# Moving four attention products of the third row of blocks from the serial opening into the first dense steps

## The chip, the cores and the metric

The program runs on one core of one Trainium2 chip. The metric is device time in microseconds (us), from one launch to its end, lower is better. The core has a matrix engine (TensorE, PE in the profile, with its weight loads as PEld), a vector engine (DVE), a scalar engine (ACT), GpSimd (POOL), SyncE (SP), which here issues most of the transfers, and 16 DMA engines. Each engine runs its own instructions in the order in which they are written and waits on semaphores for the others. SBUF is the on-chip memory, PSUM the memory that PE writes to.

## The reference, cut to what matters

Three layers follow one another: windowed attention with a bias by distance, a feed-forward layer with SiLU, and a layer of eight experts in which each token goes to one. The change lies in the first layer and in the opening of the second.

```python
def _attn_ref(q, k, v, n_global, n_local):           # q, k, v: (4, 8, 768, 64)
    scores = scale * np.matmul(q, k.transpose(0, 1, 3, 2))
    ...
    scores = np.where(keep, scores + bias, -1000000000.0)
    scores = scores - np.max(scores, axis=-1, keepdims=True)
    a = np.exp(scores)
    a = a / (np.sum(a, axis=-1, keepdims=True) + 1e-09)
    return np.matmul(a, v)                            # the "values" of this text

def _moe_ref(x, w_in, w_out):                         # x: (3072, 512)
    h = x @ w_in                                      # "up"
    g = h * (1.0 / (1.0 + np.exp(-h)))
    return (g @ w_out)                                # "down"
```

## The kernel before, in words

**Rows and units.** The 3,072 tokens are 24 rows of 128 (six per batch entry). A row has four units, each a pair of heads; unit `u` belongs to row `u // 4`. A unit goes through five stages: `score` (PE: q times k into `qk_ps`), `shift`, `exp` and `scale_probs` (DVE, ACT, DVE: the softmax), `turn` (PE transposes the probabilities into `pt_ps`), `keep_turned` (ACT copies them to a slot of `probs_t`), and `value` (PE multiplies them with the row's v in `v_w` into the one bank `o_ps`, called `notes_ps` in the rows). When a row's four values are there, `replace_x` (DVE, waits for `values_done`), `round_x` (ACT) and `rest_x` (DVE) make `x_high` and `x_low`, a high and a low part of the row. `o_ps` is single, so the first value of a row waits until `rest_x` of the row before has read it.

**Dense chunks.** Two rows are a group, and a group has 16 chunks `m`; for each PE does `up(m)` (12 matmuls of 256 columns), and two chunks later `down(m)` (6 of 512). Between them ACT does `half_tanh(m)` and `round_g(m)`, DVE `twice_silu(m)`, and POOL `rest_g(m)`, which makes `g_low`; `down(m)` waits for `g_low`. In the first group the weights are also split: a chunk's weights arrive in one of four buffers `w_raw`, ACT makes `w_high`, and DVE (even chunks) or POOL (odd ones) makes the low parts, which release the buffer for the next load.

**Order.** All engines walk over steps `n`. Steps 0 to 11 (`LEAD` is 12) are the serial opening, one unit a step with little to cover its waits. From step 12 on each step has two chunks, `m = 2(n - 12)` and the next, and `up` runs two chunks ahead. Scores come two units at a time in even steps; the four values of a row come together in every fourth step, at n = 16, 20 and so on (`valued_in`). Nothing but this written order decides what an engine does next. Steps 14 and 16, which the prediction speaks of, begin with the scores of units 14 and 15 and of units 16 and 17; step 16 has the values 12 to 15, those of row 3.

**v and the queue of SP.** `v_w` holds one row's v, so row 3's v can be loaded only when the values of row 2 (units 8 to 11) are done: the load goes in two halves, `load_v(row)` waits for `values_done` before each. SP issues all loads of q, k, v and weights one after another in the order of its own steps, and a load that waits holds up those behind it. Row 1's v lies in slots 2 and 3 of `probs_t` (`second_v`), so units before 12 use only slots 0 and 1.

Of the kernel before, what the change touches and what calls it, by code (L numbers as in the profile page):

```python
# [168 lines left out]
def attention_and_silu(nc, block, sems_ctx, first, tables, last_down, notes_ps, qk_rows, v_win, limits, beyond, weights, gate_rows,  # L169
# [6 lines left out]
    PAIRS = H // 2  # L176
# [8 lines left out]
    LEAD = 12  # L185
# [8 lines left out]
    with ExitStack() as ctx:  # L194
        def sb(name, shape, dt=F32):
            return ctx.enter_context(nc.sbuf_tensor(name, shape, dt))
# [4 lines left out]
        def sem(name):  # L201
            return sems_ctx.enter_context(nc.semaphore(name))
# [9 lines left out]
        probs_t = sb("probs_t", [P, PAIRS, 4, P])  # L212
# [34 lines left out]
        values_done = sem("values_done")  # L247
# [21 lines left out]
        def reached(eng, semaphore, value):  # L269
            if value > 0:  # L270
                eng.wait_ge(semaphore, value)

        def unit_there(u):
            return 0 <= u < UNITS
# [7 lines left out]
        def row_of(u):  # L282
            return u // PAIRS, u % PAIRS

        def keys_of(row):
            return (half, window) if row % tiles else (P // 2, P)
# [8 lines left out]
        def scored_in(n):  # L295
            return [u for u in (n, n + 1) if unit_there(u)] if n >= LEAD and n % 2 == 0 else []

        def valued_in(n):
            return [u for u in range(n - PAIRS, n) if unit_there(u) and u >= LEAD - 2] if n >= LEAD and n % PAIRS == 0 else []

        def turned_behind(m):
            n, k = LEAD + m // 2, m % 2
# [9 lines left out]
        def x_row_in(n):  # L312


            if n < LEAD:
                return row_ended(n, 3)
            return row_ended(n, 1) if n % 2 == 0 else None

        def scores_of(u):
            at = 256 if u >= LEAD and u % 2 else 0  # L320
            return qk_ps[:, :, at:at + keys_of(u // PAIRS)[1]]

        def turned_of(u):
            return probs_t[:, u % (2 if u < LEAD else PAIRS), :, :]

        def v_of(row):
            return second_v if row == 1 else v_w
# [4 lines left out]
        def row_ended(n, lag):  # L332

            u = n - lag
            return u // PAIRS if unit_there(u) and u % PAIRS == PAIRS - 1 else None
# [10 lines left out]
        def split_in(n):  # L346


            if LEAD - 4 <= n < LEAD - 2:
                return (n - LEAD + 4,)  # L350
            f = 2 * (n - LEAD + 2)
            return (f, f + 1) if LEAD - 1 <= n and f < FC else ()
# [10 lines left out]
        def rows_of(grp):  # L363

            start = sum(PER_GROUP[:grp])
            return start // E, start
# [27 lines left out]
        @block.sync  # L394
        def _(sp):
            def load_qk(row):

                reached(sp, qk_done, (row - 1) * PAIRS)
                used = P + keys_of(row)[1]
                sp.dma_start(qk_t[:, row % 2, :, 0:used], qk_rows[row, :, :, 0:used]).then_inc(qk_in[row % 2], 16)  # L400

            def load_v(row, halves=(0, 1)):


                part, _ = keys_of(row)
                for k in halves:
                    reached(sp, values_done, (row - (2 if row == 2 else 1) if row > 1 else -1) * PAIRS + (k + 1) * PAIRS // 2)
                    pairs = slice(k * PAIRS // 2, (k + 1) * PAIRS // 2)
                    sp.dma_start(v_of(row)[0:part, pairs, :, :, :], v_win[row, 0:part, pairs, :, :, :])\
                        .then_inc(v_in[row % 2 * 2 + k], 16)  # L410

            def load_weights(f):

                reached(sp, w_low_ready[f % 2], (f - RAW) // 2 + 1)
                sp.dma_start(w_raw[:, f % RAW, :], weights[f, :, :]).then_inc(w_in_sbuf[f % RAW], 16)


            sp.wait_ge(scores_ready, 2)
            load_qk(1)
            load_v(1)  # L420
            load_qk(2)
            load_v(2, (0,))
            load_weights(0)
            sp.wait_ge(bias_ready, H // 2 - 1)
            sp.wait_ge(pair_bias_ready, 1)
            load_weights(1)
            load_v(2, (1,))
            for f in range(2, RAW):
                load_weights(f)
            for n in range(UNITS + 4):  # L430
                row = row_ended(n, 0)
                if row is not None and 0 < row < ROWS - 2:
                    load_qk(row + 2)
                for f in split_in(n):
                    if f + RAW < FC:
                        load_weights(f + RAW)
                if row is not None and 1 < row < ROWS - 1:
                    load_v(row + 1)
                grp = (n - LEAD) // (FC // 2)
                if n > LEAD and (n - LEAD) % (FC // 2) == FC // 4 and 0 < grp < G - 1:  # L440

                    sp.wait_ge(dots_done, grp * GT * E)
                    sp.wait_ge(x2_stored, grp * 16)
                    chunk, _ = rows_of(grp)
                    sp.dma_start(x2[:, :, :], weights[chunk:chunk + 2, :, C * P:].rearrange("f p c -> p f c"))\
                        .then_inc(w_out_in, 16)
                if n == LEAD + FC // 2 - 2:
                    for k in range(2):
                        sp.wait_ge(w_low_ready[k], FC // 2)
                    sp.dma_start(gate_all, gate_rows.partition_broadcast(P)).then_inc(gate_all_in, 16)  # L450
# [54 lines left out]
        def _(pe):  # L505
# [29 lines left out]
            def value(u):  # L535
                row, pair = row_of(u)
                part, _ = keys_of(row)
                if pair % (PAIRS // 2) == 0:
                    pe.wait_ge(v_in[row % 2 * 2 + pair // (PAIRS // 2)], 16 * (row // 2 + 1))
                if pair == 0:  # L540
                    reached(pe, x_low_ready, row)
                pe.wait_ge(probs_t_ready, u + 1)
                for c in range(2):
                    for a in range(2):
                        last = nc.tensor.matmul(o_ps[a * D:(a + 1) * D, pair, :], v_of(row)[0:part, pair, a, c, :],
                                                turned_of(u)[0:part, a * 2 + c, :], start=c == 0, stop=c == 1)
                last.then_inc(values_done, 1)
# [46 lines left out]
            def unread_products(count):  # L594

                for _ in range(count):
                    nc.tensor.matmul(up_ps[:, 1, 256:256 + P], ident[:, :], ident[:, :], start=True, stop=True)

            for n in range(STEPS):
                if n < LEAD:  # L600


                    score(n)
                    unread_products({0: 8, 1: 3}.get(n, 0))
                    turn_last = (n - 3) % PAIRS != 0
                    if n == 2:
                        unread_products(5)
                    if n >= 2 and not turn_last:
                        turn(n - 2)
                    if n == PAIRS + 3:  # L610
                        unread_products(4)
                    if n >= 3:
                        value(n - 3)
                    if n >= 2 and turn_last:
                        turn(n - 2)
                    unread_products({2: 3, 3: 2}.get(n, 0))
                for u in scored_in(n):
                    score(u)
                for u in valued_in(n):
                    value(u)  # L620
                for m in chunks_of(n):
                    if chunk_there(m + AHEAD):
                        up(m + AHEAD)
                    if chunk_there(m) and m < LAST:
                        down(m)
                    elif chunk_there(m):
                        if m == LAST + 1:
                            pe.wait_ge(x2_ready, (G - 1) * GT)
                        last_down.products(pe, nc, downs_ahead(m))
                        last_logits(m)  # L630

                    if m == -2:
                        turn(LEAD - 2)
                        value(LEAD - 3)
                    if m == -1:
                        turn(LEAD - 1)
                    if turned_behind(m) is not None:
                        turn(turned_behind(m))
# [7 lines left out]
        def _(act):  # L646
# [9 lines left out]
            def keep_turned(u):  # L656

                row, _ = row_of(u)
                part, _ = keys_of(row)
                reached(act, values_done, u - 1 if u < LEAD + 2 else u - PAIRS + 1)  # L660
                act.wait_ge(transposed, u + 1)
                nc.scalar.activation(turned_of(u)[0:part, :, :], pt_ps[0:part, :, :], ACT.Copy)\
                    .then_inc(probs_t_ready, 1)
# [40 lines left out]
            for n in range(STEPS):  # L704
# [7 lines left out]
                row = x_row_in(n)  # L712
# [1398 lines left out]
```

## Time and profile before

| what | value |
|---|---|
| median of 3 runs | 1054.82 us (1053.95 to 1056.28) |
| the profiled execution's own time | 1054.26 us |
| its span | 1052.6 us |
| PE busy | 1029.0 us, 98% |
| DVE, ACT, POOL busy | 69%, 43%, 40% |
| clock granted to PE over the span | 0.998 of full speed |

The span is the time from the first to the last instruction on the core; the profiled execution took 1.66 us more than it. PE's share is high because its matmuls are pipelined and count as busy from issue to end. The other engines have idle time in plenty, and it costs only where PE waits for them.

### The profile page before, as it was taken

Reading aid. Unit: us, or ns where it says so; the run is one execution under the profiler, and the core shown is the slowest. Engines: PE = TensorE matmul, PEld = TensorE weight load, DVE = VectorE, ACT = ScalarE, POOL = GpSimd, SP = SyncE. Lnnn points to the kernel's source line nnn. Section 1 sums busy time; section 2 is a strip of 40 time slices with the busy share of each in tenths; the row PEclk is TensorE's granted clock in tenths of the full one; section 3 lists DMA queues with packets and bytes.
Section 4 is the critical chain, followed back from the end, with each engine's and each line's share of the span. In section 5 each row is a group of like instructions: output and inputs, shape, how many; then the busy total and the mean of one; then the engine's idle time right before and its main releaser. Section 6 shows DMA issues by size and latency. Waiting matters only on the chain. (4 is left out here: it accounts for less than half of the span.)

```text
span 1052.6 us, 20243 instructions
## 1 busy us (share of the span) xinstructions
PE 1029.0 (98%) x7331; PEld 888.2 (84%) x7331; DVE 721.7 (69%) x2535; ACT 457.1 (43%) x1170; POOL 425.2 (40%) x474
## 2 busy tenths in 40 slices
PE   8899999999999999999999999998999999999998
PEld 7688888888888888888888888986778878878997
DVE  6764767777777777877777786765767868766210
ACT  5775444444544454444444443320434334334442
POOL 1363222222222222222222134312776777678773
PEclk9999999999999999999999999999999999999999
DMA  6653212222221222122222111003154254335320
GB/s 185 225 205 125 75 60 77 77 70 66 78 67 54 76 77 67 59 70 65 71 77 78 39 50 31 21 1 140 72 213 156 96 198 178 126 138 191 140 110 31
DMA packets 25827, 103.41 MB, mean 98 GB/s; under 512 B 3024, under 2 KB 5072, under 8 KB 23536
## 3 DMA queue, kind: packets, MB, share of 16 engines
q0 software_dynamic: 9824, 58.99, 15.6%
q1 hardware_dynamic: 15904, 43.13, 12.4%
q8 instruction: 59, 0.97, 0.4%
q14 instruction: 40, 0.33, 0.1%
HBM read 89.52 MB, written 12.85 MB: 97 GB/s over the span
## 5 line engine op out<-in xcount | busy, mean ns | idle before, releaser
L476 POOL TENSOR_TENSOR g_low<-g,g_high 128x256 fp32r<-128x256 f32 x176 | 142.6, 811 | 433.0 <-ACT g_high L690 433.0
L576 PE MATMUL up_ps<-x_high,w_high 128*128 128x256 f32 x768 | 227.7, 297 | 0.0
L576 PE MATMUL up_ps<-x_low,w_high 128*128 128x256 f32 x768 | 215.3, 280 | 0.0
L576 PE MATMUL up_ps<-x_high,w_in_low 128*128 128x256 f32 x768 | 215.2, 280 | 0.0
L690 ACT ACTIVATE g_high<-g 128x256 fp32r<-128x256 f32 x176 | 73.5, 418 | 211.1 <-DVE g L872 126.6
L576 PEld LDWEIGHTS up_ps<-x_high,w_high 128*128 128x128 f32 x768 | 144.6, 188 | 12.0 <-issue 9.1
L872 DVE SCALAR_TENSOR_TENSOR g<-g,up_ps 128x256 f32<-128x256 f32 x192 | 79.9, 416 | 98.2 <-ACT g L682 97.8
L576 PEld LDWEIGHTS up_ps<-x_low,w_high 128*128 128x128 f32 x768 | 144.7, 188 | 2.2
L576 PEld LDWEIGHTS up_ps<-x_high,w_in_low 128*128 128x128 f32 x768 | 144.4, 188 | 0.0
L830 DVE CUSTOM_DVE_ANT_0 product<-x,w_raw 128x512 bf16<-128x512 f32 x176 | 141.2, 802 | 3.0
L590 PE MATMUL down_ps<-w_high,g_high 128*128 128x512 f32 x352 | 138.8, 394 | 0.9 <-POOL g_low L476 0.9
L590 PE MATMUL down_ps<-w_high,g_low 128*128 128x512 f32 x352 | 139.4, 396 | 0.0
L590 PE MATMUL down_ps<-w_out_low,g_high 128*128 128x512 f32 x352 | 138.8, 394 | 0.0
L842 DVE CUSTOM_DVE_ANT_0 product<-x,w_raw 128x512 bf16<-128x512 f32 x128 | 103.9, 811 | 33.9 <-DMA x<-weights 31.9
L652 ACT ACTIVATE probs<-probs,neg_max 128x232 f32<-128x232 f32 (+1 forms) x184 | 85.1, 464 | 47.0 <-DVE neg_max L770 46.9
L682 ACT ACTIVATE g<-up_ps 128x256 f32<-128x256 f32 x192 | 72.9, 380 | 74.7 <-PE up_ps L576 55.3
L1537 POOL TENSOR_TENSOR w_low<-w_raw,w_high 128x512 fp32r<-128x512 f32 x64 | 82.0, 1292 | 46.1 <-ACT w_high L1740 43.9
L1676 PE MATMUL eup_ps<-ex_high,w_high 128*128 128x384 f32 x256 | 91.6, 358 | 1.1 <-DVE ex_low L1991 1.1
L1676 PE MATMUL eup_ps<-ex_high,w_low 128*128 128x384 f32 x256 | 86.1, 336 | 0.0
L1676 PE MATMUL eup_ps<-ex_low,w_high 128*128 128x384 f32 x256 | 86.1, 336 | 0.0
L1522 POOL TENSOR_TENSOR w_low<-w_raw,w_high 128x512 fp32r<-128x512 f32 x64 | 80.1, 1289 | 2.6 <-ACT w_high L1733 2.5
L590 PEld LDWEIGHTS down_ps<-w_high,g_low 128*128 128x128 f32 x352 | 66.1, 188 | 15.3
(244 smaller groups left out, 1984.0 us busy)
## 6 DMA issues: line engine op xcount, KB each, us to landing
qk_t<-qk_rows SPq DMA_DIRECT2D x20, 720.0 KB, 4.2
v_w<-v_win SPq DMA_DIRECT2D x38, 232.0 KB
w_raw<-weights SPq DMA_DIRECT2D x16, 512.0 KB, 4.6
x_rest<-x_any POOLq DMA_DIRECT2D x24, 256.0 KB, 2.9
x_rows<-x POOLq DMA_DIRECT2D x12, 512.0 KB, 3.2
x<-weights SPq DMA_DIRECT2D x10, 512.0 KB, 3.6
w_raw<-gate_rows SPq DMA_DIRECT2D x1, 2048.0 KB, 8.0
qk_t<-qk_rows SPq DMA_DIRECT2D x3, 512.0 KB, 3.9
```

The source lines that it names most:

```text
L476: pool.tensor_tensor(g_low_of(u), g[:, u % 2, :], g_high_of(u).bitcast(F32), ALU.subtract)\
L576: last = nc.tensor.matmul(up_ps[:, u % 2, 0:GT * P], a[:, f, w], x[:, grp % 2, c, :], start=k == 0, stop=k == 3 * C - 1)
L590: last = nc.tensor.matmul(down_ps[:, t, :], a[:, m % 2, t * P:(t + 1) * P], x[:, f, :], start=f == 0 and k == 0, stop=f == FC - 1 and k == 2)
L652: nc.scalar.activation(probs_of(u)[:, a, 0:width], probs_of(u)[:, a, 0:width], ACT.Exp, bias=neg_max[:, u % 3, a:a + 1], scale=-1.0, accum ...
L682: nc.scalar.activation(g[:, u % 2, :], up_ps[:, u % 2, 0:GT * P], ACT.Tanh, scale=0.5)\
L690: nc.scalar.activation(g_high_of(u), g[:, u % 2, :], ACT.Copy).then_inc(g_high_ready, 1)
L830: v.tensor_tensor_reduce(out=product[:, :], in0=x2[:, t, :], in1=gate_all[:, e, :], scale=1.0, scalar=0.0, op0=ALU.mult, op1=ALU.add, accu ...
L842: v.tensor_tensor_reduce(out=product[:, :], in0=x2[:, k // E - chunk, :], in1=gate_all[:, k % E, :], scale=0.5, scalar=0.0, op0=ALU.mult, ...
L872: v.scalar_tensor_tensor(g[:, u % 2, :], g[:, u % 2, :], 1.0, up_ps[:, u % 2, 0:GT * P], ALU.add, ALU.mult).then_inc(g_ready, 1)
L1522: pool.tensor_tensor(w1_low[:, f, :], w1_raw[:, p % 2, f, :], w1_high[:, f, :].bitcast(F32), ALU.subtract).then_inc(w1_low_ready, 1)
L1537: pool.tensor_tensor(w2_low[:, f, :], w2_raw[:, f, :], w2_high[:, f, :].bitcast(F32), ALU.subtract).then_inc(w2_low_ready, 1)
L1676: last = nc.tensor.matmul(up_ps[:, f % UP_BANKS, 0:CAP], w[:, f, c * P:(c + 1) * P], x[:, c, :], start=k == 0, stop=k == 3 * C - 1)
```

## The change

In the opening, the values of row 2 (units 8 to 11) were computed at steps 11, 11, 12 and 12, each soon after its probabilities were turned. They are now computed two at a time in the dense steps: units 8 and 9 at step 12, units 10 and 11 at step 14. What makes `x_high` and `x_low` of row 2 follows in step 14 instead of step 12. Units 8 to 11 use all four slots of `probs_t`, so that each has its own. SP's load of v for row 3 moves from step 11 to step 14, behind the weights that are issued there, since the values it waits for now come later.

```diff
         def valued_in(n):
-            return [u for u in range(n - PAIRS, n) if unit_there(u) and u >= LEAD - 2] if n >= LEAD and n % PAIRS == 0 else []
+            if n in (LEAD, LEAD + 2):
+
+                return [n - PAIRS, n - PAIRS + 1]
+            return [u for u in range(n - PAIRS, n) if unit_there(u)] if n > LEAD and n % PAIRS == 0 else []
...
-            if n < LEAD:
+            if n < LEAD or n == LEAD + 2:
                 return row_ended(n, 3)
-            return row_ended(n, 1) if n % 2 == 0 else None
+            return row_ended(n, 1) if n > LEAD and n % 2 == 0 else None
...
-            return probs_t[:, u % (2 if u < LEAD else PAIRS), :, :]
+            return probs_t[:, u % (2 if u < LEAD - PAIRS else PAIRS), :, :]
...
                 for f in split_in(n):
                     if f + RAW < FC:
                         load_weights(f + RAW)
+
+                row = row_ended(n, 3) if n == LEAD + 2 else row if n > LEAD else None
                 if row is not None and 1 < row < ROWS - 1:
                     load_v(row + 1)
...
-                    if n >= 3:
+                    if 3 <= n < LEAD - 1:
                         value(n - 3)
...
                     if m == -2:
                         turn(LEAD - 2)
-                        value(LEAD - 3)
...
-                reached(act, values_done, u - 1 if u < LEAD + 2 else u - PAIRS + 1)
+                reached(act, values_done, u - 1 if u < LEAD - 2 else max(u - PAIRS + 1, 2 * PAIRS))
                 act.wait_ge(transposed, u + 1)
```

Line numbers behind the first edit grow by 3 to 5. In the rows below, `value` is L545 before and L550 after, `up` L576 and L581, `load_v` L409 and L412, `load_weights` L415 and L418, `load_qk` L400 and L403.

PE, from the turning of unit 9 to the `up` of chunk 2, before, with what the first instruction of each piece waits for (`up` of chunks 0 and 1 stand behind the first two values; rows left out are the other matmuls of each piece and the turns of units 10 and 11):

```order
L531 MATMUL pt_ps<-ident,probs 116x128 [waits probs_t_ready,scaled]
...
L545 MATMUL notes_ps<-probs_t,v_w 64x128 [waits probs_t_ready,x_low_ready,v_in0]
...
L576 MATMUL up_ps<-x_high,w_high 128x256 [waits w_low_ready0,x_low_ready]
...
L545 MATMUL notes_ps<-probs_t,v_w 64x128 [waits probs_t_ready]
...
L576 MATMUL up_ps<-x_high,w_high 128x256 [waits w_low_ready1]
...
L518 MATMUL qk_ps<-qk_t 128x232 [waits scores_ready,qk_in1]
...
L545 MATMUL notes_ps<-probs_t,v_w 64x128 [waits probs_t_ready,v_in1]
...
L576 MATMUL up_ps<-x_high,w_high 128x256 [waits g_ready,w_low_ready0]
```

The scores of units 12 to 15 and the values behind them on PE in the changed kernel, in the same manner (the first four rows open step 12, the last four step 14):

```order
L523 MATMUL qk_ps<-qk_t 128x232 [waits scores_ready,qk_in1]
...
L550 MATMUL notes_ps<-probs_t,v_w 64x128 [waits probs_t_ready,x_low_ready,v_in0]
...
L550 MATMUL notes_ps<-probs_t,v_w 64x128 [waits probs_t_ready]
...
L581 MATMUL up_ps<-x_high,w_high 128x256 [waits g_ready,w_low_ready0]
...
L523 MATMUL qk_ps<-qk_t 128x232 [waits scores_ready]
...
L550 MATMUL notes_ps<-probs_t,v_w 64x128 [waits probs_t_ready,v_in1]
...
L550 MATMUL notes_ps<-probs_t,v_w 64x128 [waits probs_t_ready]
...
L581 MATMUL up_ps<-x_high,w_high 128x256 [waits g_ready,w_low_ready0]
```

No value stands between a turn and an `up` any more; two values follow the scores in step 12, and two more in step 14, where none stood.

SP, from the load of row 3's q and k on, before (the x6 are the weights of chunks 8 to 13):

```order
L400 DMA qk_t<-qk_rows 128x1440
L415 DMA w_raw<-weights 128x1024 x2
L400 DMA qk_t<-qk_rows 128x1440
L415 DMA w_raw<-weights 128x1024 x2
L409 DMA v_w<-v_win 116x512 x2
L415 DMA w_raw<-weights 128x1024 x6
L400 DMA qk_t<-qk_rows 128x1440
L415 DMA w_raw<-weights 128x1024 x2
```

SP in the changed kernel, the same place:

```order
L403 DMA qk_t<-qk_rows 128x1440
L418 DMA w_raw<-weights 128x1024 x2
L403 DMA qk_t<-qk_rows 128x1440
L418 DMA w_raw<-weights 128x1024 x8
L412 DMA v_w<-v_win 116x512 x2
L403 DMA qk_t<-qk_rows 128x1440
L418 DMA w_raw<-weights 128x1024 x2
```

The two halves of row 3's v (116 partitions of 512 elements each) stood ahead of the weights of chunks 8 to 13 and now stand behind them, between the weights of chunk 13 and the q and k of row 5.

DVE in step 14 of the changed kernel, from `replace_x` of row 2 to the low parts of the weights of chunk 8:

```order
L806 COPY_PREDICATED notes_ps<-beyond,x_rest 128x512
L785 TENSOR_SCALAR inv<-sums 128x2
L787 RECIPROCAL inv<-inv 128x2
L790 TENSOR_SCALAR probs<-probs,inv 128x232 x2
L785 TENSOR_SCALAR inv<-sums 128x2
L787 RECIPROCAL inv<-inv 128x2
L790 TENSOR_SCALAR probs<-probs,inv 128x232 x2
L813 TENSOR_TENSOR x_low<-notes_ps,x_high 128x4x128
L876 SCALAR_TENSOR_TENSOR g<-g,up_ps 128x256
L798 TENSOR_TENSOR w_in_low<-w_raw,w_high 128x512
```

The first row and the `x_low` row stood in step 12 before; in step 14 they are new, both ahead of `g` of chunk 6.

## Rows read from the trace of the kernel before

**Rows 1.** The page: busy time of the engines, share of the span, instructions

```profile
PE 1029.0 (98%) x7331; PEld 888.2 (84%) x7331; DVE 721.7 (69%) x2535; ACT 457.1 (43%) x1170; POOL 425.2 (40%) x474
```

**Rows 2.** Busy time by stretch: length, busy PE, PEld, DVE, ACT, POOL, clock, DMA share, GB/s

```profile
35.00:44.00 9.00, 7.43 (x72) 5.97 (x70) 6.62 (x26) 6.27 (x16) 2.00 (x2) 1.00 0.71 254
44.00:60.00 16.00, 16.00 (x108) 13.89 (x105) 10.62 (x30) 11.48 (x28) 11.23 (x11) 1.00 0.60 182
60.00:80.00 20.00, 20.00 (x155) 17.64 (x154) 12.29 (x36) 14.46 (x32) 11.71 (x12) 1.00 0.52 191
...
110.00:640.00 530.00, 529.33 (x3889) 461.46 (x3888) 401.69 (x1322) 242.66 (x697) 136.65 (x178) 1.00 0.20 66
```

**Rows 3.** Timeline of PE, steps 11 and 12: start, length, instruction, idle before it

```profile
34.86 0.66 PE L545 MATMUL notes_ps<-probs_t,v_w 116*64 116x128 f32 x8 [0.78 <-issue]
...
37.56 0.65 PE L531 MATMUL pt_ps<-ident,probs 128*116 128x128 f32 x4 [0.43 <-DVE probs L786]
...
43.56 0.66 PE L545 MATMUL notes_ps<-probs_t,v_w 116*64 116x128 f32 x8 [1.14 <-ACT probs_t L662]
...
44.14 0.39 PE L576 MATMUL up_ps<-x_high,w_high 128*128 128x256 f32 x1
...
45.70 0.50 PE L590 MATMUL down_ps<-w_high,g_high 128*128 128x512 f32 x1
```

**Rows 4.** Timeline of POOL from 44.3 us: `rest_g` of chunk 0

```profile
44.47 1.18 POOL L476 TENSOR_TENSOR g_low<-g,g_high 128x256 fp32r<-128x256 f32 x1
```

**Rows 5.** Timeline of PE at the start of step 14, then of step 16

```profile
56.59 1.05 PE L518 MATMUL qk_ps<-qk_t 64*128 64x232 f32 x8
57.58 0.39 PE L576 MATMUL up_ps<-x_high,w_high 128*128 128x256 f32 x1
...
69.89 1.05 PE L518 MATMUL qk_ps<-qk_t 64*128 64x232 f32 x8
70.87 1.97 PE L545 MATMUL notes_ps<-probs_t,v_w 116*64 116x128 f32 x32
72.77 0.38 PE L576 MATMUL up_ps<-x_high,w_high 128*128 128x256 f32 x1
```

**Rows 6.** Timeline of DVE and POOL, steps 14 and 16

```profile
61.34 0.42 DVE L872 SCALAR_TENSOR_TENSOR g<-g,up_ps 128x256 f32<-128x256 f32 x1
...
64.77 1.29 POOL L463 TENSOR_TENSOR w_out_low<-w_raw,w_high 128x512 fp32r<-128x512 f32 x1
...
72.95 0.70 DVE L802 COPY_PREDICATED notes_ps<-beyond,x_rest 128x512 f32<-128x512 int32 x1 [0.50 <-PE notes_ps L545]
...
76.17 0.41 DVE L872 SCALAR_TENSOR_TENSOR g<-g,up_ps 128x256 f32<-128x256 f32 x1
```

**Rows 7.** Timeline of SP: issues of weights, q and k, and v

```profile
49.99 16.42 SPq L415 DMA_DIRECT2D w_raw<-weights  x6
66.45 0.43 SPq L400 DMA_DIRECT2D qk_t<-qk_rows  x1
...
72.00 1.15 SPq L409 DMA_DIRECT2D v_w<-v_win  x2
```

**Rows 8.** The weights' transfers of 512 KB between 38 and 80 us

```profile
DMA to landing us min/median/max: 3.4/4.0/5.1
```

**Rows 9.** DMA from 72 to 82 us in 40 slices, then 74.8 to 80.5 us

```profile
DMA  9988999961122222222222252222200000000000
...
DMA  2114122122232222222227222222222200000000
...
q1 hardware_dynamic: 210, 0.41, 20.3%
```

**Rows 10.** PE around its only drop of clock: timeline, then columns as Rows 2

```profile
727.66 0.75 PE L1619 MATMUL route_ps<-ids,one_hot 128*32 128x24 bf16 x24 [2.76 <-issue]
...
725.00:730.00 5.00, 2.34 (x32) 2.34 (x33) 1.46 (x8) 0.00 (x0) 2.34 (x4) 0.94 0.76 246
730.00:735.00 5.00, 5.00 (x24) 5.00 (x23) 2.81 (x11) 0.00 (x0) 3.74 (x4) 0.72 0.95 392
```

## The prediction

> **What bounds the kernel now.** The page comes first: PE is busy for 1029.0 us, 98% of the span, the next engine, DVE, for 69% [rows 1]. The busy time by stretch then shows where PE has slack: from 44 to 80 us PE is busy all the time, and from 110 to 640 us it lacks 0.67 us of 530 [rows 2]. So whatever moves PE's work in the opening shifts all that follows by the same amount, up or down, and nothing behind it can take a delay back. The question is when PE gets through step 16, where the order of its work is again the same in both kernels.
>
> The timeline of PE in steps 11 and 12 has three waits: 0.78 us before the value of unit 8 (it waits for `x_low` of row 1, since `o_ps` is single), 0.43 us before the turn of unit 10, and 1.14 us before the value of unit 11, whose turned probabilities ACT has not yet copied. Then `up` of chunk 2 starts at 44.14 us and `down` of chunk 0 at 45.70 us [rows 3].
>
> **What the change removes.** Four values leave the stretch before 44.14 us, 0.66 us of PE for each [rows 3], and with them the wait of 1.14 us. But each saving ends at the next wait. `up` of chunk 0 waits for the same `x_low` as the value did, so it starts about 0.6 us earlier; the turn of unit 10 then waits for DVE, which is untouched, and starts at 37.56 us as before. From there the value of unit 9 (0.6 us) and the 1.14 us fall away, and units 8 and 9 stand where 10 and 11 stood, with no wait. `up` of chunk 2 therefore starts some 1.7 us earlier, near 42.4 us. Behind it stands `down` of chunk 0, which waits for `g_low` from POOL: that instruction runs from 44.47 to 44.47 + 1.18 = 45.65 us, and `down` starts at 45.70 us [rows 3, 4]. What POOL does before hangs on ACT and DVE, which wait for none of the removed values. So nearly all of the 1.7 us turns into a wait for POOL. Bounds: at least 0 (POOL as now); at most 0.45 us, if the 1.18 us shrink to 0.73 us, where DVE's work beside it changes. I take 0.1 us gained, near the lower end, since DVE will scale probabilities beside it instead of replacing x.
>
> **What it adds.** Two values in step 14. From the scores to the first `up` it takes 57.58 - 56.59 = 0.99 us there now, and 72.77 - 69.89 = 2.88 us in step 16, where four values stand between [rows 5]. Two values are half of the difference, 0.95 us, on a PE with no idle time. The other two only fill the place of units 10 and 11.
>
> **What it moves, and what is late next.** The load of row 3's v is the step that I take to decide. Before, it was issued in step 12. Now SP issues it in step 14 behind the weights of chunk 13. That load waits until POOL has made the low parts of chunk 9's weights, at 64.77 + 1.29 = 66.06 us [rows 6], and the row after it on SP (q and k of row 5) shows the queue free at 66.45 us [rows 7]. So v would be issued at 66.45 us, plus what DVE and POOL are later. They are later, because `replace_x`, 0.70 us, and `x_low` now stand ahead of `g` of chunk 6. In step 14 now, `g` starts 61.34 - 56.59 = 4.75 us after the scores; in step 16, with four values and both instructions, 76.17 - 69.89 = 6.28 us [rows 5, 6]. The difference of 1.53 us holds four values; two values less give between 0.6 and 1.5 us, and I take 1.0. Issue of v: 66.45 + 1.0 = 67.45 us, the second half some 0.4 us behind.
>
> How long does it take? By size alone it would be quick: 512 KB of weights land in 3.4 to 5.1 us [rows 8], and each half of v has 232 KB. The next load of v says otherwise. It was issued from 72.00 us [rows 7]. In the DMA view from 72 us the engines are nearly all busy until about 74.2 us with what was queued before, and then one fifth of them until about 79.5 us; from 74.8 us on the queue has 210 packets, no more than 20.3% of 16 engines, that is three to four of them, and the last slice with traffic ends near 79.8 us [rows 9]. So both halves together have landed some 7.8 us after the issue, and the first, taken as half of the 5.6 us from 74.2 us, about 5 us after it. The Trainium skill (DMA: Bandwidth & Descriptors, Why a DMA increments its semaphore by 16 and not by 1) says that a transfer is split over the largest number of engines, at most 16, that divides its slowest dimension. For 116 partitions that makes 4 engines; the trace agrees with its 20.3%.
>
> When does PE want it? The values of units 12 to 15 start at 70.87 us [rows 5]; shifted by -0.1 + 0.95 that is 71.72 us. The first half lands at 67.45 + 5 = 72.45 us or later: a wait of 0.7 us, up to 1.6 us if it takes 5.9. Unit 14 needs the second half, which PE reached at 70.87 + 0.98 = 71.85 us before. It lands at 67.45 + 7.8 = 75.25 us at the earliest, so PE is 3.4 us later there than before. Something comes on top: the semaphore, and row 5's q and k and the x of POOL's queue, which are in flight at the same time, while almost nothing ran beside the load that I read. Bounds for the second half: 7.8 us (as read) and 9.3 us (1.5 us on top, a fifth more). I take 8.6 us. PE is then at 67.45 + 8.6 - 71.85 = 4.2 us later than before, and as the order is the same from there, it stays so.
>
> **The sum.** -0.1 (opening) + 0.95 (two values) + 3.35 (waits for the halves of v) = +4.2 us. Against the profiled execution's own 1054.26 us that is 1058.5 us; the median of the runs shown is 0.56 us above that execution, so 1059.0 us for the median. The cost of all other edits is nothing: the four slots add no instruction, and ACT's new wait for 8 values is fulfilled before each copy. If SP's load of v came in time, that cover would make the sum +0.85 us.
>
> **Rivals.**
> - *v lands in time.* Then no wait stands in step 16: +0.4 to +1.3 us, 1055.2 to 1056.1, which 0.2% (2.1 us, about what a measurement tells from no change) doesn't tell from the kernel before. For it speak the 3.4 to 5.1 us of the larger weights [rows 8]. It is decided by the second half: it must land within 71.72 + 0.98 - 67.45 = 5.2 us of the issue. Against it stand the 7.8 us of the next load. This is the rival on the other side. If the wait of 1.14 us also paid off in full because POOL came earlier, it would be -1.6 + 0.95 = -0.65 us, still within 0.2%; faster than that needs something that no row shows.
> - *v is late, but by little.* SP gets to the load earlier (the 1.0 us does not come about, since DVE has idle time in step 14), and the halves run beside each other. PE would be later by 75.25 - 1.0 - 71.85 = 2.4 us: 1057.2.
> - *The wait costs clock as well.* PE's granted clock fell below full speed in the stretch from 725 us on, in which PE had been idle for 2.76 us before 727.66 us: 0.94 in the first five microseconds, 0.72 in the next [rows 10]. That is 0.3 + 1.4 = 1.7 us lost. In step 16 two waits of 1 to 2.5 us stand with only one short piece of work between; if the clock fell there as well, the sum would be 4.2 + 1.7 = +5.9 us, 1060.7. Against it: from 35 to 44 us PE was idle for 1.57 of 9 us and kept the full clock [rows 2], and in the changed kernel it is busy from 46 us to the first of these waits.
>
> **How the numbers follow.** Late v as summed, with its bounds +3.3 to +5: 0.63. Late by little, +1 to +3.3: 0.17, half of it over 2.1 us. Clock as well, +5 to +7: 0.06. v in time: 0.12. Faster by another way: 0.02. So slower by over 0.2% has 0.63 + 0.08 + 0.06 = 0.77, within 0.2% 0.12 + 0.09 = 0.21, faster 0.02. The range goes from 1055.8 (v nearly in time) to 1060.4 us; the forecast's own is 1058.1 to 1059.8.
>
> **What the changed profile would show.** Right: PE waits in `down` of chunk 0 for POOL's `g_low`, which still ends near 45.6 us; two values of about 1 us in step 14; SP issues v near 67.5 us; and PE waits twice at L550 near 72 us, first for one transfer of v, about 1 us, then for the other, about 2.4 us; from there on each piece stands 4.2 us later than before. Wrong: no wait at L550 in step 16 (the transfer is quicker or earlier than I read), or `down` of chunk 0 well before 45.2 us (POOL was not what it waited for), or a wait in steps 14 and 15, where `up` of chunks 8 and 9 needs the low parts that DVE and POOL now make a microsecond later.

## The result and the profile after

The changed kernel takes 1064.45 us (median of 4 runs, 1062.69 to 1065.81), the kernel before 1055.32 us (4 runs): ratio 1.0093, 95% interval 1.0081 to 1.0105, so 9.1 us slower. The forecast was 1059.0 us with a range up to 1060.4. The profiled execution took 1065.81 us, span 1064.1 us.

The timeline of PE in the changed kernel, from the turn of unit 9 to the scores of step 18; it answers to [rows 3, 5] (start, length, instruction, idle before it and what ended it):

```profile
33.75 0.65 PE L536 MATMUL pt_ps<-ident,probs 128*116 128x128 f32 x4 [0.83 <-DVE probs L790]
35.14 0.39 PE L581 MATMUL up_ps<-x_high,w_high 128*128 128x256 f32 x1 [0.74 <-DVE x_low L813]
37.88 1.11 PE L536 MATMUL pt_ps<-ident,probs 128*116 128x128 f32 x4 [0.65 <-DVE probs L790]
...
43.63 1.09 PE L550 MATMUL notes_ps<-probs_t,v_w 116*64 116x128 f32 x16
...
56.97 1.05 PE L523 MATMUL qk_ps<-qk_t 64*128 64x232 f32 x8
57.95 1.09 PE L550 MATMUL notes_ps<-probs_t,v_w 116*64 116x128 f32 x16
...
71.27 1.05 PE L523 MATMUL qk_ps<-qk_t 64*128 64x232 f32 x8
74.96 1.10 PE L550 MATMUL notes_ps<-probs_t,v_w 116*64 116x128 f32 x16 [2.63 <-DMA v_w<-v_win]
79.20 1.97 PE L550 MATMUL notes_ps<-probs_t,v_w 116*64 116x128 f32 x16 [3.15 <-DMA v_w<-v_win]
...
94.70 1.05 PE L523 MATMUL qk_ps<-qk_t 64*128 64x232 f32 x8
```

In step 16 PE waits twice for a half of row 3's v, 2.63 and 3.15 us. The last value row shows one thing more: its 16 matmuls take 1.97 us, those of the row ahead of it 1.10 us. The busy time by stretch of the changed kernel says why (columns as in [rows 2]; the seventh number is the granted clock):

```profile
33.00:37.00 4.00, 2.51 (x16) 2.21 (x16) 3.26 (x11) 1.73 (x5) 0.54 (x1) 0.90 0.65 230
37.00:43.00 6.00, 5.35 (x26) 4.74 (x26) 3.68 (x11) 4.58 (x12) 0.68 (x1) 0.50 0.87 311
43.00:60.00 17.00, 17.00 (x136) 14.61 (x133) 9.88 (x33) 12.16 (x30) 11.76 (x12) 1.00 0.44 145
77.00:78.00 1.00, 0.00 (x0) 0.00 (x0) 0.00 (x0) 0.00 (x0) 0.00 (x0) 0.58 0.99 220
78.00:84.00 6.00, 4.80 (x29) 4.47 (x30) 2.46 (x10) 0.60 (x1) 0.00 (x0) 0.50 0.29 108
84.00:90.00 6.00, 6.00 (x42) 5.42 (x41) 3.19 (x5) 4.10 (x7) 3.73 (x4) 1.00 0.15 57
```

The clock fell to half speed (1.2 instead of 2.4 GHz) twice: in the opening, and again while PE idled in the second wait for v, from where it stayed low until 84 us.

SP in the changed kernel, answering to [rows 7]: v is issued at 67.78 us.

```profile
67.41 0.33 SPq L418 DMA_DIRECT2D w_raw<-weights  x1
67.78 0.73 SPq L412 DMA_DIRECT2D v_w<-v_win  x2
68.55 0.35 SPq L403 DMA_DIRECT2D qk_t<-qk_rows  x1
69.98 2.92 SPq L418 DMA_DIRECT2D w_raw<-weights  x2
```

**Where the 9.65 us up to step 18 are** (starts of the same instructions on PE in both profiled executions; the scores of step 18 start at 85.05 us before):

| from | to | before | after | difference |
|---|---|---|---|---|
| launch | turn of unit 9 | 33.43 | 33.75 | +0.32 |
| turn of unit 9 | scores of step 14 | 23.16 | 23.22 | +0.06 |
| scores of step 14 | scores of step 16 | 13.30 | 14.30 | +1.00 |
| scores of step 16 | scores of step 18 | 15.16 | 23.43 | +8.27 |

In the last line 2.63 + 3.15 = 5.78 us are waits. Of the other 2.49 us, 2.30 us are the clock: from the start of unit 14's values to the scores of step 18 PE takes 94.70 - 79.20 = 15.50 us, before 85.05 - 71.85 = 13.20 us, for it works at half speed from 79.20 to 84.0 us and does 2.4 us of work in these 4.8 us. The last 0.19 us stand around the waits.

The first line is outside the change. The +0.06 us of the second line are two things that cancel: with the clock at full speed the changed opening takes 22.71 us to the scores of step 14 (e3, e5b and e9 below take 22.71 to 22.72), 0.45 us less than before, and the half speed in this execution costs 0.5 us. So here `up` of chunk 2 starts 44.66 - 33.75 = 10.91 us after the turn of unit 9, no earlier than before (10.71 us), and `down` of chunk 0 follows it without a wait:

```profile
44.66 0.39 PE L581 MATMUL up_ps<-x_high,w_high 128*128 128x256 f32 x1
...
46.18 0.40 PE L595 MATMUL down_ps<-w_high,g_high 128*128 128x512 f32 x1
```

From step 18 to the routing of tokens both kernels take the same (642.6 and 642.7 us), and further on the changed one's profiled execution loses another 1.7 us of its span, most of it near 745 us, by a fall of the clock that the kernel before has too, elsewhere.

### The profile page after: what moved, and what is told of

Read it like the earlier page. It is cut to its first block and busy times, and to the rows that moved or that the text cites. A ratio compares the mean times of both kernels' runs of the same rounds, so it can differ in the third digit from the quotient of the medians.

```text
span 1064.1 us, 20243 instructions
## 1 busy us (share of the span) xinstructions
PE 1033.8 (97%) x7331; PEld 893.0 (84%) x7331; DVE 722.0 (68%) x2535; ACT 457.2 (43%) x1170; POOL 424.0 (40%) x474
## 5 line engine op out<-in xcount | busy, mean ns | idle before, releaser
L581 PE MATMUL up_ps<-x_high,w_high 128*128 128x256 f32 x768 | 229.1, 298 | 0.7 <-DVE x_low L813 0.7
L581 PE MATMUL up_ps<-x_low,w_high 128*128 128x256 f32 x768 | 216.5, 282 | 0.0
L581 PE MATMUL up_ps<-x_high,w_in_low 128*128 128x256 f32 x768 | 216.5, 282 | 0.0
L581 PEld LDWEIGHTS up_ps<-x_high,w_high 128*128 128x128 f32 x768 | 145.8, 190 | 12.6 <-issue 9.1
L581 PEld LDWEIGHTS up_ps<-x_low,w_high 128*128 128x128 f32 x768 | 146.0, 190 | 2.2
L581 PEld LDWEIGHTS up_ps<-x_high,w_in_low 128*128 128x128 f32 x768 | 145.7, 190 | 0.0
```

The lines of the kernel that those rows point to most:

```text
L581: last = nc.tensor.matmul(up_ps[:, u % 2, 0:GT * P], a[:, f, w], x[:, grp % 2, c, :], start=k == 0, stop=k == 3 * C - 1)
```

## The experiments

Each was timed in turns with the kernel before on the same chip. The kernel before had medians of 1053.52 to 1055.32 us in these sessions, so kernels of different rows are compared by their ratios, not by their medians. "Waits" is what PE waited for v in step 16, "clock" whether it fell below full speed at or behind these waits, both in the profiled execution.

| kernel | median us | ratio to before, 95% | waits, us | clock |
|---|---|---|---|---|
| changed kernel | 1064.45 | 1.0093 (1.0081 to 1.0105) | 2.63 + 3.15 | fell |
| e1: v issued early | 1055.03 | 1.0007 (0.9995 to 1.002) | none | full |
| e2: only the load moved | 1064.2 | 1.0086 (1.0069 to 1.0103) | 3.47 + 2.80 | fell |
| e3: v as 112 + 4 partitions | 1055.75 | 1.0014 (1.0003 to 1.0026) | 0.50 | full |
| e4: opening filled | 1062.88 | 1.0071 (1.0054 to 1.0088) | 3.14 + 2.34 | fell |
| e5b: no SP transfer issued behind v | 1063.44 | 1.0091 (1.0075 to 1.0106) | 3.05 + 0.62 | fell |
| e9: nothing issued behind v | 1062.33 | 1.0064 (1.0044 to 1.0084) | 1.86 + 1.89 | fell |
| e11: waits filled with work | 1060.35 | 1.0063 (1.005 to 1.0077) | 1.32 + 0.21 | full |
| e6b: e1, filled, POOL's order | 1052.41 | 0.9983 (0.9974 to 0.9992) | none | full |
| e10: e6b without the filling | 1053.28 | 0.9987 (0.9979 to 0.9996) | none | full |
| e7b: before, POOL's order, values | 1053.25 | 0.9991 (0.9982 to 1.0) | none | full |
| e8b: before, POOL's order | 1054.23 | 1.0004 (0.9994 to 1.0013) | none | full |

### e1: the load of v at its earliest places

```diff
+                if n in (LEAD, LEAD + 2):
+                    load_v(3, ((n - LEAD) // 2,))
                 for f in split_in(n):
                     if f + RAW < FC:
                         load_weights(f + RAW)
-                row = row_ended(n, 3) if n == LEAD + 2 else row if n > LEAD else None
-                if row is not None and 1 < row < ROWS - 1:
+                if n > LEAD and row is not None and row < ROWS - 1:
                     load_v(row + 1)
```

> The changed kernel, but SP issues the first half of row 3's v in step 12 ahead of the weights of chunks 8 and 9, and the second half in step 14 ahead of the weights of chunks 12 and 13. The values stay where the change put them. Theory A (the load of v is late because of its place on SP): the waits of 2.63 and 3.15 us in step 16 vanish, and with them the clock fall at 77.5 us; what is left is 0.5 us in the opening and 0.9 us for two values, so 1.4 us over the kernel before, 1056.7 us, up to 1.7 us more if the later clock fall stays long. Theory B (the moved values and the clock in the opening cost it): the time stays over 1060 us.

Measured: 1055.03 us, 0.7 us over before, an interval that includes no change, and 1.7 us less than Theory A gave. Its 0.5 us for the opening are not there: from the turn of unit 9 to the scores of step 14 it takes 56.56 - 33.36 = 23.20 us, 23.16 before. The timeline of PE in step 16 has no wait, and all 32 value matmuls in one piece as in the kernel before:

```profile
56.56 1.05 PE L523 MATMUL qk_ps<-qk_t 64*128 64x232 f32 x8
57.55 1.09 PE L550 MATMUL notes_ps<-probs_t,v_w 116*64 116x128 f32 x16
...
70.88 1.05 PE L523 MATMUL qk_ps<-qk_t 64*128 64x232 f32 x8
71.86 1.97 PE L550 MATMUL notes_ps<-probs_t,v_w 116*64 116x128 f32 x32
```

From the scores of step 14 to those of step 16 it takes 14.32 us, 1.02 over the 13.30 us of before: the two added values, and nothing else. So nearly the whole loss of the change hangs on where SP issues two loads. Theory B falls.

### e2: the load's new place alone, in the kernel before

```diff
+                row = row_ended(n, 3) if n == LEAD + 2 else row if n > LEAD else None
                 if row is not None and 1 < row < ROWS - 1:
                     load_v(row + 1)
```

> The kernel before with one part of the change: SP issues both halves of row 3's v in step 14 behind the weights of chunk 13. Values, slots and the engines' order are as before. Theory A: v is issued at 66.4 us and its second half lands some 11.4 us later, at 77.8 us, where PE wants it at 71.9 us: about 6 us of waits in step 16, and 2 us by the clock behind them, 1063 us. The opening keeps its full clock. Theory B: 1055 to 1057 us.

Measured: 1064.2 us, ratio 1.0086. With not one value moved it is as slow as the changed kernel. v is issued at 67.09 us here, its second half is there 12.0 us later, and the opening kept its full clock, as expected. The waits in step 16 of this kernel:

```profile
75.02 1.31 PE L546 MATMUL notes_ps<-probs_t,v_w 116*64 116x128 f32 x16 [3.47 <-DMA v_w<-v_win]
79.13 1.97 PE L546 MATMUL notes_ps<-probs_t,v_w 116*64 116x128 f32 x16 [2.80 <-DMA v_w<-v_win]
```

### e3: row 3's v split into 112 and 4 partitions

```diff
-                    sp.dma_start(v_of(row)[0:part, pairs, :, :, :], v_win[row, 0:part, pairs, :, :, :])\
-                        .then_inc(v_in[row % 2 * 2 + k], 16)
+                    for rows in (slice(0, 112), slice(112, part)) if row == 3 else (slice(0, part),):
+                        sp.dma_start(v_of(row)[rows, pairs, :, :, :], v_win[row, rows, pairs, :, :, :])\
+                            .then_inc(v_in[row % 2 * 2 + k], 16)
...
-                    pe.wait_ge(v_in[row % 2 * 2 + pair // (PAIRS // 2)], 16 * (row // 2 + 1))
+                    pe.wait_ge(v_in[row % 2 * 2 + pair // (PAIRS // 2)],
+                               16 * (row // 2 + 1 + (row % 2 and row >= 3)))
```

The second part makes PE wait for both transfers of a half.

> The changed kernel, but each half of row 3's v goes as two transfers, one of 112 partitions and one of 4, in the same place on SP. Theory A1 (the load is slow because 116 partitions go over four DMA engines): the halves land within 3 to 5 us of the issue at 67.8 us, so PE waits less than 1 us in step 16, 1057 to 1058 us. Theory A2 (it is slow because q, k, x and weights are in flight with it on the same engines): the waits stay over 4 us and the time over 1061 us.

Measured: 1055.75 us, 1.4 us over the kernel before, less than the 1057 to 1058 us of Theory A1. The late place stays, the issue is at 67.58 us (67.78 in the changed kernel), and still only 0.5 us of waits are left:

```profile
72.08 1.10 PE L552 MATMUL notes_ps<-probs_t,v_w 116*64 116x128 f32 x16
73.68 1.09 PE L552 MATMUL notes_ps<-probs_t,v_w 116*64 116x128 f32 x16 [0.50 <-DMA v_w<-v_win]
```

The second half, the last of four transfers issued between 67.58 and 69.1 us, is there at 73.68 us, 6.1 us after the first issue instead of 79.20 - 67.78 = 11.4 us; that is longer than the 3 to 5 us expected, but nearly short enough. So two things make the loss together, the late issue and the narrow transfer; to mend either takes nearly all of it away. The same kernel shows the opening at full clock, as the prediction had it: `up` of chunk 2 starts 8.83 us after the turn of unit 9 (34.07 us), 1.88 us earlier than before, and `down` of chunk 0 waits for POOL.

```profile
45.91 0.50 PE L597 MATMUL down_ps<-w_high,g_high 128*128 128x512 f32 x1 [1.33 <-POOL g_low L482]
```

### e4: unread products in the opening

```diff
+                    if n == LEAD - 1:
+                        unread_products(2)
...
                     if m == -2:
+                        unread_products(3)
                         turn(LEAD - 2)
```

> The changed kernel with five unread products of 128 by 128 on PE in the opening, two behind the turn of unit 9 and three ahead of the turn of unit 10, where PE waits anyway. Theory C (the clock fell to half speed at 36.6 us because PE lost work in the opening when the values went): the clock stays full up to the waits in step 16, up of chunk 2 starts near 42.7 instead of 44.66 us, and down of chunk 0 near 46.0 us, held by POOL's g_low; the time falls by 0.3 to 0.5 us only, since the waits of step 16 stay, 1064 us. If the clock falls all the same, it is not these 1.3 us of work.

Measured: 1062.88 us, and the clock was full up to step 16; `down` of chunk 0 started at 45.30 us. But this settles less than it seems: e3, e5b, e9, e10 and e11, which have no such products, kept their clock in the opening too, the profiled executions of the changed kernel and of e1 did not, and neither did that of e8b, in which no value is moved. That the removed values are what lowers the clock there is not shown; it falls in some executions. It costs 0.5 us: to the scores of step 14 the changed kernel and e1 take 23.22 and 23.20 us from the turn of unit 9, e3 and this kernel 22.71 and 22.72.

This kernel shows one thing more: its clock fell near 74.5 us, in the first wait, before any value of step 16, and in e2 and e5b it fell while the first values ran. The second wait was not needed for it.

### e5b and e9: nothing issued behind v

Both are the changed kernel with SP held back in step 15:

```diff
+                if n == LEAD + 3:
+                    sp.wait_ge(v_in[2], 32)
+                    sp.wait_ge(v_in[3], 32)
                 if row is not None and 0 < row < ROWS - 2:
                     load_qk(row + 2)
```

> The changed kernel, but SP waits in step 15 until both halves of row 3's v have landed before it issues q and k of row 5 and the weights of chunks 14 and 15. Only POOL's transfer of x stays beside v. Theory A2 (half of the forecast's error is that the other transfers slow v's four engines): the second half lands about 8 to 9 us after the issue instead of 11.4, the two waits at the values of step 16 sum to about 3 to 3.5 us instead of 5.8, and the time is 1061 to 1062 us. Theory A1 (v takes as long by itself): the waits stay at 5.8 us, 1064 us. A new wait could come at the up of chunks 14 and 15, whose weights are 6 us later; I expect none, since ACT rounds them only in step 17.

e9 also issues POOL's x for row 3 earlier:

```diff
-                if row is not None:
+                if n == LEAD + 2:
+                    load_rest(3)
+                elif row is not None and row != 3:
                     load_rest(row)
```

> As e5b_v_alone, and in addition POOL issues its transfer of x for row 3 at the start of step 14, near 60 us, so that it is over before v is issued at 67.5 us: nothing else is in flight beside row 3's v. Theory A2: both halves land within 7.8 to 8.3 us, as the load of row 4 in the kernel before did, the first after 5 us: PE waits near 72.5 us for under 0.7 us and then for 1.5 to 2 us, 2.2 to 2.7 us in all. If the clock keeps its full speed over these shorter waits, the time is 3.5 us above before, 1057.8 us; if it falls as it did in e5b_v_alone, 1061 us. Theory A1: waits of 3.7 us as in e5b_v_alone.

Measured: the waits are 3.67 us in e5b and 3.75 us in e9, some 2.1 us less than in the changed kernel. Up to the scores of step 18 that is what PE gains: 58.96 and 58.81 us from the turn of unit 9, 60.95 in the changed kernel. The whole times hardly follow, 1063.44 and 1062.33 us (ratios 1.0091 and 1.0064), both above what was expected. No new wait came at the `up` of chunks 14 and 15. Three views of e9 follow: the last issues of SP ahead of the wait, with the time that the weights took to land; PE in step 16; and DMA from 69 to 79 us.

```profile
67.27 0.33 SPq L418 DMA_DIRECT2D w_raw<-weights  x1
67.64 0.73 SPq L412 DMA_DIRECT2D v_w<-v_win  x2
...
w_raw<-weights SPq DMA_DIRECT2D x1, 512.0 KB, 4.1
```

```profile
74.05 1.09 PE L555 MATMUL notes_ps<-probs_t,v_w 116*64 116x128 f32 x16 [1.86 <-DMA v_w<-v_win]
77.03 1.97 PE L555 MATMUL notes_ps<-probs_t,v_w 116*64 116x128 f32 x16 [1.89 <-DMA v_w<-v_win]
```

```profile
DMA  9797553241222321222223222221000000009957
```

The second half is there only at 77.03 us, 9.4 us after the first issue at 67.64 us, though nothing is issued behind it. It is not alone from the start: the weights of chunk 13, 512 KB, were issued 0.37 us ahead of it and landed 4.1 us after their issue, near 71.4 us. The DMA row shows the engines busy by half or more until 70.5 us and then about one in five of them until 76.5 us, as in [rows 9]; PE starts 0.5 us behind these last data. So of the 9.4 us some 2.9 go by with the weights ahead still filling the engines, 6.0 on a few engines, and 0.5 to the start on PE.

What is issued behind v adds 11.4 - 9.4 = 2.0 us. Of this, 1.6 us are SP's q, k and weights (e5b: 77.30 - 67.50 = 9.8 us) and 0.4 us POOL's x, which delays the first half more, by 1.2 us (7.6 us after the issue in e5b, 6.4 in e9). These differences are of single executions; among the four with the same transfers behind v (the changed kernel, e2, e4, e11) the second half came 11.4 to 12.0 us after the first issue. Theory A2 is right that the transfers beside v slow it, but they are the smaller part, and its 7.8 to 8.3 us for e9 are wrong; the waits of e9 are those of Theory A1. In both kernels the clock fell near 76 us and came back near 82.5 us, so that 5 us or more of its low stretch lay on dense work.

### e11: the waits filled with unread work

```diff
                 for u in valued_in(n):
+                    if n == LEAD + PAIRS and u % 2 == 0:
+                        pe.wait_ge(x_low_ready, 3)
+                        for _ in range(8 if u == LEAD else 10):
+                            nc.tensor.matmul(o_ps[:, u % PAIRS, :], ident[:, :], ident[:, :], start=True, stop=True)
                     value(u)
```

> The changed kernel with unread products of 128 by 128 on PE in step 16, where it waits for v: 8 ahead of the value of unit 12 (about 2.1 us) and 10 ahead of that of unit 14 (2.6 us), written to the places of o_ps that those values then overwrite. v lands when it did, near 74.9 and 79.2 us, so the values start when they did. Theory K (the clock falls at 77.5 us because PE idles in the waits, and costs 2.5 us more behind them): the clock stays full, and the time falls by 2.5 us against the changed kernel, 1062 us. If the clock falls all the same or the time stays at 1064.5 us, the waits are not what lowers it.

Measured: 1060.35 us. The timeline of PE in step 16 and the stretches around it:

```profile
72.27 2.05 PE L628 MATMUL notes_ps<-ident 128*128 128x128 f32 x16
75.64 1.09 PE L550 MATMUL notes_ps<-probs_t,v_w 116*64 116x128 f32 x16 [1.32 <-DMA v_w<-v_win]
76.67 2.50 PE L628 MATMUL notes_ps<-ident 128*128 128x128 f32 x20
79.37 1.09 PE L550 MATMUL notes_ps<-probs_t,v_w 116*64 116x128 f32 x16 [0.21 <-DMA v_w<-v_win]
```

```profile
70.00:80.00 10.00, 8.47 (x78) 7.09 (x78) 1.78 (x9) 2.79 (x10) 3.20 (x3) 1.00 0.90 238
80.00:90.00 10.00, 10.00 (x74) 8.93 (x70) 5.88 (x16) 6.25 (x12) 4.41 (x4) 1.00 0.20 76
```

The values of unit 14 start when they did (79.37 and 79.20 us), but now at full clock, and the scores of step 18 come at 92.72 instead of 94.70 us. Counted from the turn of unit 9 (34.23 us here) that is 58.49 instead of 60.95 us, 2.46 us less, for the 2.5 us expected. Of these, 2.15 us lie behind the start of unit 14's values (13.35 instead of 15.50 us); 0.3 us come from ahead of it, since this execution also kept its clock in the opening. The whole kernel gained more, 0.0030 by the ratios, which is 3.2 us; in the profiled executions 3.3 us of it lie behind step 18, where the routing's fall of clock came 10 us earlier than in the changed kernel. Why is open.

### e6b, e10, e7b, e8b: what the opening can give

The prediction had the opening's gain end at POOL's `g_low`. These kernels put it ahead of the low parts of chunk 3's weights, for which POOL waits anyway (`rest_w` in step 11 moves behind the first `rest_g`):

```diff
-                if n < LEAD:
+                if n < LEAD - 1:
                     for f in rests:
                         rest_w(f)
...
-                    if n >= LEAD and m % 2 == 0:
+                    if n >= LEAD - 1 and m % 2 == 0:
                         for f in rests:
                             rest_w(f)
```

e6b is e1 with this and e4's products, e10 e1 with this alone. e8b is the kernel before with this alone, and e7b adds to it that the values of units 10 and 11 stand behind `up` of chunk 2.

> The changed kernel with v's halves issued as in e1_v_early, the unread products of e4_filled, and POOL's g_low of chunk 0 ahead of the low parts of chunk 3's weights in step 11. Theory P (the gain of the opening ends at POOL's g_low): down of chunk 0 starts near 44.0 instead of 45.3 us, so the time falls by 1.3 us against e1_v_early with a full clock: 1053.7 us, that is 0.6 us below the kernel before, since two values in step 14 still cost 0.9 us. Theory Q (something else stands behind it, such as the low parts of chunk 3 for up of chunk 3): 1055 us.

> As e6b_early_filled_pool without the five unread products. If the gain of that kernel comes from POOL's order alone, the time is its 1052.4 us. If the clock falls in the opening without the unread products, up of chunk 2 starts near 44.5 instead of 42.6 us and nothing of POOL's order is gained: 1054.3 us.

> The kernel before with two edits: POOL's g_low of chunk 0 ahead of the low parts of chunk 3's weights, and the values of units 10 and 11 in step 12 behind up of chunk 2 instead of ahead of it. Theory P: the 1.14 us wait for ACT's copy is covered by up of chunk 2, down of chunk 0 starts near 44.4 instead of 45.7 us, and nothing is added later: 1.3 us below the kernel before, 1053.0 us. Theory Q: 1054.3 us.

> The kernel before with POOL's g_low of chunk 0 ahead of the low parts of chunk 3's weights, alone. In the kernel before up of chunk 2 ends just when that g_low is ready, so both theories expect the time of before within 0.1%: 1054.3 us.

Measured: e6b 1052.41 us, ratio 0.9983 (0.9974 to 0.9992), the fastest of all. Its `down` of chunk 0:

```profile
44.18 0.39 PE L595 MATMUL down_ps<-w_high,g_high 128*128 128x512 f32 x1
```

That is 10.34 us after the turn of unit 9 (33.84 us), against 12.27 us in the kernel before, 1.9 us gained; the two values in step 14 give 1.0 back. Against e4, which has the same opening at full clock without POOL's new order (45.30 - 33.46 = 11.84 us), it is 1.50 us, for the 1.3 us of Theory P. The ratio gives 1.8 us below the kernel before (0.8 to 2.7), where it claimed 0.6 and the timeline of PE up to step 16 shows 1.0. e10 has 0.9987 (0.9979 to 0.9996), which doesn't differ from e6b: the gain comes from POOL's order, and whether the products add to it is not told by these runs. e7b, 0.9991 (0.9982 to 1.0), falls short of its 1.3 us. Its `down` of chunk 0 did start 1.31 us earlier (10.96 us after the turn of unit 9), but then `up` of chunk 4 met the next bound, DVE's low parts of that chunk's weights:

```profile
50.44 0.38 PE L576 MATMUL up_ps<-x_high,w_high 128*128 128x256 f32 x1 [0.68 <-DVE w_out_low L798]
```

DVE is no later with them than before: they end 16.5 us after the turn of unit 9 in both kernels. PE only comes early to them, and 0.35 us are left of the gain at the scores of step 14. e8b, 1.0004, shows that POOL's order alone gives nothing.

## Why the prediction was wrong

**Right.** What bounds the kernel and that no later slack takes a delay back: from step 18 to the routing the two kernels take the same time within 0.1 us. The two added values: 0.95 forecast, 1.00 measured. The issue of v: 67.45 forecast, 67.78 measured; counted from the scores of step 14 the load of chunk 13's weights ahead of it came 0.95 us later than before, 1.0 forecast. That PE would wait twice in step 16, first for one half and then for the other, and that about four engines carry the transfer.

**Right by luck: the opening.** -0.1 us was forecast and +0.06 measured, but not in the way written. In the changed kernel's profile PE does not wait in `down` of chunk 0 for POOL's `g_low`, one of the signs named for being right, because the clock was at half speed and `up` of chunk 2 late. With the full clock (e3) the mechanism is as written, with a wait of 1.33 us for `g_low`; the gain is then 0.45 us, the upper bound of the forecast and not its 0.1 us, for POOL's `g_low` took 0.71 us there instead of 1.18.

**Wrong in size: the landing of v.** "I take 8.6 us" for the second half, with 9.3 us as the bound; it was 11.4 us. Two parts of that step failed. The load read for it, that of row 4, was taken from its last data in the DMA view, and its queue stood otherwise: e9 shows 9.4 us for row 3's load with nothing issued behind it, so the 7.8 us were 1.6 us short. Of these, 0.5 us pass between the last data and the start on PE, and about 0.7 us because the weights ahead filled the engines for 2.9 us after the issue, not 2.2. And what came on top from the transfers behind it was put at 0.8, at most 1.5 us, where e9 against the changed kernel shows 2.0 us. So the waits were 5.78 us, not 3.35.

**Wrong in the likeliest case: the clock.** The rival in which "the wait costs clock as well" had a chance of 0.06 and 1.7 us; it happened, and cost 2.3 of the 2.49 us that the table has beside the waits. The clock fell in all five profiled kernels that waited between 3.67 and 6.27 us in step 16, and stayed in the two that waited 0.50 and 1.53 us. The reasons against it, that the opening's waits had left the clock alone and that PE was dense before, did not hold: here PE stood idle for 1.86 to 3.47 us in the first wait, behind 20 us and more of dense work. e11 shows the cause: with v as late and the waits filled, the clock stays and 2.15 us come back behind unit 14's values.

The sum by the measured terms is 0.06 + 1.00 + 5.78 + 2.49 = 9.3 us, against 9.1 us between the medians. The sum as forecast, +4.2 us, lacks 2.4 us of wait, and the 2.5 us of the clock, which it left out as an unlikely rival.

## What to carry to other kernels

When an edit moves work that frees a buffer, follow the load that waits for the buffer: where it now stands in its queue, and how long it takes by a load of the same shape with the same transfers ahead of it and behind it, from issue to the use that waits for it, not by its bytes or its last data. In this kernel waits that summed to 3.7 to 6.3 us, on a PE that was otherwise busy, lowered the clock in five profiled kernels of five, so a forecast of such waits carries that price as the likely case, not as a rare one. And before moving work out of a serial stretch, look at what its next instruction waits for: here the values and the 1.14 us were worth 0.45 us at most until another engine's order was changed too, and then DVE was next.

## What the hardware showed that was not expected

- Two transfers of 116 partitions, 232 KB each, were there 9.4 us after the first issue with nothing issued behind them (e9), and after 11.4 us with other traffic; as 112 + 4 partitions they were there after 6.1 us, beside the other traffic (e3). The Trainium skill (DMA: Bandwidth & Descriptors, Why a DMA increments its semaphore by 16 and not by 1) has the number of engines as the largest divisor up to 16, which gives 4 for 116 and 16 for 112. The 24.9% of 16 engines that the queue of e9 used from 73 to 75 us agree with 4; that 112 partitions go over 16 no row shows by itself, but the 6.1 us fit it.
- The granted clock fell in the opening in some executions and not in others of nearly the same program: in the profiled ones of the changed kernel, e1 and e8b, and in none of the other ten. Its low stretch in the routing came at different places between 720 and 760 us. What decides either is open. The intervals in the table reach about 1 us and more to either side, so smaller differences between kernels are not told apart here.
